# Per-row weights' norm moved into a diagonal product, the steps after it one slot later, and loads spread over the slots of an unrolled attention and FFN program

## What is computed

```python
scores = scale * np.matmul(q, k.transpose(0, 1, 3, 2))
kth = np.partition(scores, -top_k, axis=-1)[..., -top_k:-top_k + 1]   # top_k = 32
scores = np.where(scores >= kth, scores, -1000000000.0)
attn = np.exp(scores - np.max(scores, axis=-1, keepdims=True))
attn = attn / (np.sum(attn, axis=-1, keepdims=True) + 1e-09)
x = np.matmul(attn, v)                      # rows of 8 heads x 64
h = x @ w_in;  y = (h - np.tanh(h)) @ w_out            # first FFN, 512 -> 2048 -> 512
h = y @ w_in2; g = np.where(h > 0, h, np.exp(np.minimum(h, 0)) - 1); out = g @ w_out2
```

## Time and profile before

| | |
|---|---|
| median of 3 runs | 1504.14 us |
| the profiled execution: its own time | 1504.16 us |
| its span, first to last instruction | 1502.3 us |
| mean granted TensorE clock | 0.911 |
| busy: PE, PEld, DVE, ACT, POOL | 1220.8, 1016.0, 849.9, 773.3, 623.1 us |
| chain that ended last | PE 36%, POOL 28%, issue 26%, ACT 4%, DVE 2% |

### The profile page before, as it was taken

The page is one execution under the profiler, slowest core; times in us unless marked ns, Lnnn a source line. Parts: engine busy times, 40 slices in busy tenths (PEclk is TensorE's granted clock), DMA queues, the critical chain, the costliest instruction groups (busy, mean ns, idle before and its releaser), DMA issues.

```text
span 1502.3 us, 21851 instructions
## 1 busy us (share of the span) xinstructions
PE 1220.8 (81%) x7448; PEld 1016.0 (68%) x7448; DVE 849.9 (57%) x1796; ACT 773.3 (51%) x1792; POOL 623.1 (41%) x968
## 2 busy tenths in 40 slices
PE   1455577878877878888678888788999999999998
PEld 1344456657666667777566777677778888888887
DVE  4667776757878657877667788740442222222221
ACT  3456556656667656766665666653532222222221
POOL 1256535555545545544555545444522222222222
PEclk9855679989999879999898999999999999999999
DMA  8200002100001110001110000002410100101000
GB/s 264 74 12 12 7 20 60 43 25 16 12 26 51 51 34 15 12 26 31 52 55 9 27 13 14 18 29 71 148 63 0 56 1 21 36 1 42 1 29 14
DMA packets 45853, 55.93 MB, mean 37 GB/s; under 512 B 9136, under 2 KB 26544, under 8 KB 45744
## 3 DMA queue, kind: packets, MB, share of 16 engines
q1 hardware_dynamic: 45744, 54.55, 11.7%
HBM read 45.09 MB, written 9.44 MB: 36 GB/s over the span
## 4 chain that ended last, share of the span: by engine, by line
PE 36%; POOL 28%; issue 26%; ACT 4%; DVE 2%; SPq 2%; DMA 1%; POOLq 0%; ACTq 0%
PE ps L544 13%; PE ps L527 13%; POOL gT_lo L907 6%; POOL scores L898 6%; POOL gT_raw L902 5%; POOL qT_lo L861 3%; PE ps L497 3%; PE ps L464 2%; POOL kT_hi_over_lo L868 2%; POOL weight_sum_eps L893 2%; PE ps L447 1%; POOL xT_lo L880 1%; POOL exp_bias L886 1%; PE ps L483 1%; PE ps L436 1%
## 5 line engine op out<-in xcount | busy, mean ns | idle before, releaser
L776 DVE MAX8 best<-work 128x8 f32<-128x576 f32 x432 | 309.2, 744 | 0.2
L447 PE MATMUL ps<-ident,scores 128*128 128x128 f32 x576 | 107.9, 318 | 206.9 <-POOL scores L898 206.8
L447 PEld LDWEIGHTS ps<-ident,scores 128*128 128x128 f32 x576 | 74.8, 161 | 225.5 <-POOL scores L898 225.4
L950 POOL TENSOR_TENSOR elu_lo<-elu_h,elu_hi 128x512 fp32r<-128x512 f32 x72 | 92.9, 1290 | 317.6 <-ACT elu_hi L580 317.6
L785 DVE MATCH_REPLACE8 work<-best,work 128x576 f32<-128x576 f32 x288 | 214.0, 743 | 0.0
L907 POOL TENSOR_TENSOR gT_lo<-gT_raw,gT_hi 128x256 fp32r<-128x256 f32 x144 | 109.8, 762 | 200.3 <-ACT gT_hi L580 200.3
L836 DVE TENSOR_SCALAR exp_h<-exp_h 128x512 f32<-128x512 f32 x72 | 30.7, 427 | 269.6 <-ACT exp_h L728 269.6
L902 POOL TENSOR_TENSOR gT_raw<-gT_raw,tanh_h 128x256 f32<-128x256 f32 x144 | 106.1, 737 | 179.2 <-ACT tanh_h L647 178.8
L580 ACT ACTIVATE weights_T<-ps 128x512 f32<-128x512 f32 (+1 forms) x288 | 107.9, 428 | 131.5 <-PE ps L448 131.5
L483 PE MATMUL ps<-xT_hi,w_in_hi 128*128 128x256 f32 x576 | 165.8, 288 | 1.6 <-ACT weights_T L580 1.6
L602 ACT ACTIVATE scores<-ps 128x576 f32<-128x576 f32 x144 | 92.2, 641 | 143.0 <-PE ps L437 142.9
(11 more groups left out here) (73 smaller groups left out, 3083.7 us busy)
## 6 DMA issues: line engine op xcount, KB each, us to landing
kT_raw<-kT SPq DMA_DIRECT2D x64, 144.0 KB, 2.8
qT_raw<-qT SPq DMA_DIRECT2D x128, 64.0 KB, 2.2
w_in_raw<-w_in SPq DMA_DIRECT2D x8, 1024.0 KB, 6.6
w_out_raw<-w_out SPq DMA_DIRECT2D x8, 1024.0 KB, 7.2
ffn_rows<-y_rows SPq DMA_DIRECT2D x18, 256.0 KB, 2.0
v_rows<-v SPq DMA_DIRECT2D x16, 256.0 KB, 3.0
rows<-ffn_rows SPq DMA_DIRECT2D x4, 1024.0 KB, 5.9
out<-out_rows SPq DMA_DIRECT2D x16, 256.0 KB, 2.5
```

The lines of the kernel that those rows point to most:

```text
L447: pe.transpose(ps[:, B_TURN, c * P:(c + 1) * P], w[:, c * P:(c + 1) * P], ident[:, :])
L776: nc.vector.max(best[:, u.t % 3, 1 + n * EIGHT:1 + (n + 1) * EIGHT], src).then_inc(done, 1)
```

## The change

- `norm` is gone. POOL multiplies a 128x128 matrix of ones on the diagonal (kept as bytes) by the inverse (`set_diag`), in the same memory as the identity, and `turn_weights` is an ordinary product of the weights with that diagonal matrix.
- `invert`, `set_diag`, the turn and `copy_turned` come one slot later, in u+3. `invert` stands behind the first MAX8 of its slot. `attend` stands behind the turn of the same slot and ahead of `y_step`. `copy_scores` still reuses the buffer of the unit 4 before it, so it now waits for the turn of its own slot.
- The order within ScalarE's and POOL's slots is written anew: `copy_x` first and `copy_scores`, `copy_turned` behind `tanh_step`; on POOL `difference` first and `sum_eps`, `biases` behind the low parts.
- The weights' loads are issued one in each second slot (2 to 16), each after a wait on `scored`. At the start only one q and one k are split ahead of the slots; the low parts of the first batch's other k come to POOL, in two halves as all k do; the slots of k for later batches change.
- `y_rows` gets a buffer for each of 4 tiles, in the memory of the high part of x; both copies of a group's end stand together, and an x tile waits for its buffer's save.
- For the 21 chunks from EARLY = 123 on (they run when the attention is over) DVE makes the difference straight from PSUM, and the low part, in place of ScalarE's copy and two POOL operations.
- Of the second FFN's weights a quarter is split before it and three quarters beside its first 12 steps (before: three quarters and a quarter).

The diff's core. Renames, semaphores, sizes and waits with the same meaning are left out.

```diff
@@ -95,6 +95,8 @@
+    EARLY = sum(s <= T + 2 for s in h_slot)
@@ -115,12 +117,14 @@
+    K_AFTER = (1, 2, 4, 6, 8, 9, 10, 12)
+    K_FIRST = {-1: (1, 2), 0: (3,), 1: (4,), 2: (5,), 3: (6,), 4: (7,)}
-            k_slot[first + 1 + h * 11 // 7] = (b, h)
+            k_slot[first + K_AFTER[h]] = (b, h)
@@ -156,21 +160,24 @@
+        diag = ident
+        ones_at = place("diagonal_ones", [P, P], U8)
+        y_rows = place("y_rows", [P, KC, RING * P], offset=xt_at)
-        y_rows = place("y_rows", [P, DM])
...
@@ -256,7 +265,7 @@
         def rest_bank(u):
-            return B_H + next_chunk(u.t + 3) % 2
+            return B_H + (next_chunk(u.t + 3) + 1) % 2
@@ -268,6 +277,8 @@
+        w_load_slot = {2 * i + 2: i for i in range(2 * FB)}
@@ -285,13 +296,14 @@
-        w2_in_at, w2_out_at = {}, {}
-        for fb in range(FB - 1):
-            for n in range(CPB):
-                w2_in_at.setdefault(4 * fb + 6 + n // 2, []).append(fb * KC + n)
-                w2_out_at.setdefault(4 * fb + 8 + n // 2, []).append(fb * CPB + n)
-        w2_in_late = {f: [(FB - 1) * KC + 2 * f, (FB - 1) * KC + 2 * f + 1] for f in (0, 1)}
-        w2_out_late = {f: [(FB - 1) * CPB + 2 * f - 4, (FB - 1) * CPB + 2 * f - 3] for f in (2, 3)}
+        w2_in_at = {6: (0, 1), 7: (2, 3)}
+        w2_out_at = {8: (0, 1), 9: (2, 3)}
+        w2_in_late, w2_out_late = {}, {}
+        for fb in range(1, FB):
+            for n in (0, 1):
+                c = fb * CPB + 2 * n
+                w2_in_late[4 * fb - 4 + n] = (c, c + 1)
+                w2_out_late[4 * fb - 2 + n] = (c, c + 1)
@@ -334,6 +346,7 @@
             def load_weights(i):
+                sp.wait_ge(scored, 2 * i + 3)
@@ -374,8 +388,6 @@
-            for i in range(2 * FB):
-                load_weights(i)
@@ -383,18 +395,22 @@
+                if s in w_load_slot:
+                    load_weights(w_load_slot[s])
...
@@ -439,13 +456,16 @@
             def turn_weights(u):
-                pe.wait_ge(normed, u.t + 1)
+                pe.wait_ge(diag_set, u.t + 1)
-                after(pe, tanh_done, next_chunk(u.t + 3) - 1)
+                after(pe, tanh_done, next_chunk(u.t + 3))
-                    pe.transpose(ps[:, B_TURN, c * P:(c + 1) * P], w[:, c * P:(c + 1) * P], ident[:, :])
-                pe.transpose(ps[0:REST, rest_bank(u), REST_AT:BANK], w[:, FULL * P:S], ident[:, :]).then_inc(turned, 1)
+                    pe.matmul(ps[:, B_TURN, c * P:(c + 1) * P], w[:, c * P:(c + 1) * P], diag[:, :],
+                              start=True, stop=True)
+                pe.matmul(ps[0:REST, rest_bank(u), REST_AT:BANK], w[:, FULL * P:S], diag[:, :],
+                          start=True, stop=True).then_inc(turned, 1)
@@ -475,7 +495,8 @@
-                after(pe, turned_copied, min(h_slot[i] - 3, T - 1) + 1)
+                after(pe, g_done_late, i - 1 - EARLY)
+                after(pe, turned_copied, min(h_slot[i] - 4, T - 1) + 1)
@@ -486,12 +507,15 @@
             def y_step(i):
-                pe.wait_ge(g_split, i + 1)
-                if f == 0:
-                    after(pe, y_copied, g * GN)
+                if i < EARLY:
+                    pe.wait_ge(g_split, i + 1)
+                else:
+                    pe.wait_ge(g_split_late, i + 1 - EARLY)
+                    if f == 0 and g > 0:
+                        pe.wait_ge(y_copied, (g - 1) * GN + j + 1)
@@ -545,17 +570,16 @@
...
             for s in range(-1, LAST + 1):
-                done, old, new = unit(s - 3), unit(s - 2), unit(s + 1)
-                if done and done.ends_pair:
-                    attend(done)
+                exped_u, new = unit(s - 3), unit(s + 1)
-                if old:
-                    turn_weights(old)
+                if exped_u:
+                    turn_weights(exped_u)
+                if exped_u and exped_u.ends_pair:
+                    attend(exped_u)
...
@@ -636,24 +660,28 @@
             def x_high_part(tile):
-                after(sc_e, h_done, ((seq_of[tile] - RING) // GN + 1) * FC)
+                after(sc_e, y_saved[seq_of[tile] % RING], seq_of[tile] // RING * DMA)
             def tanh_step(i):
-                high(gt_raw[:, i % 2, :], ps[:, B_H + i % 2, 0:N])
+                if i < EARLY:
+                    high(gt_raw[:, i % 2, :], ps[:, B_H + i % 2, 0:N])
...
             def copy_y(g, j):
-                after(sc_e, y_saved, (g * GN + j) * DMA)
-                high(y_rows[:, :], ps[:, B_Y + j, :]).then_inc(y_copied, 1)
+                high(y_rows[:, :, x_columns(tiles[g * GN + j])], ps[:, B_Y + j, :].rearrange("p (c n) -> p c n", c=KC)
+                     ).then_inc(y_copied, 1)
@@ -671,43 +699,42 @@
-            for n in range(QRING):
-                q_high_part(n)
-                if n == 0:
-                    k_high_part(0, 0)
-                k_high_part(0, n + 1)
+            q_high_part(0)
+            k_high_part(0, 0)
             for s in range(-1, LAST + 1):
-                new, old, done = unit(s + 1), unit(s - 2), unit(s - 3)
+                new, old, exped_u, done = unit(s + 1), unit(s - 2), unit(s - 3), unit(s - 4)
+                if done and done.ends_pair:
+                    copy_x(done)
-                if new:
-                    copy_scores(new)
-                if y_in.get(s - 1, 0) % FC == FC - 1:
-                    copy_y(y_in[s - 1] // FC, 0)
-                    copy_x(done)
-                for n in q_load_slot.get(s - 1, ()):
+                if y_in.get(s - 1, 0) % FC == FC - 1:
+                    for j in range(GN):
+                        copy_y(y_in[s - 1] // FC, j)
+                if s in h_in:
+                    tanh_step(h_in[s])
+                if new:
+                    copy_scores(new)
+                if exped_u:
+                    copy_turned(exped_u)
+                if 0 <= s < QRING - 1:
+                    q_high_part(s + 1)
+                for n in q_load_slot.get(s, ()):
-                if 0 <= s and s + 4 < H:
-                    k_high_part(0, s + 4)
+                for h in K_FIRST.get(s, ()):
+                    k_high_part(0, h)
-                if s in h_in:
-                    tanh_step(h_in[s])
-                if old:
-                    copy_turned(old)
-                if y_in.get(s - 1, 0) % FC == FC - 1:
-                    copy_y(y_in[s - 1] // FC, 1)
@@ -728,6 +755,9 @@
+                    if g == 0 and f == 0:
+                        for n in range(RING):
+                            sc_e.wait_ge(y_saved[n], (TILES - n + RING - 1) // RING * DMA)
@@ -788,32 +818,45 @@
 ...
+            def difference(i):
+                ve.wait_ge(tanh_done, i + 1)
+                after(ve, y_done, i - 1)
+                nc.vector.tensor_tensor(gt_raw[:, i % 2, :], ps[:, B_H + i % 2, 0:N], gt_tanh[:, i % 2, :], ALU.subtract
+                                        ).then_inc(g_done_late, 1)
+            def g_low_part(i):
+                ve.wait_ge(g_high, i + 1)
+                nc.vector.tensor_tensor(gt_lo[:, i % 2, :], gt_raw[:, i % 2, :], gt_hi[:, i % 2, :], ALU.subtract
+                                        ).then_inc(g_split_late, 1)
-            for h in range(PAIRS):
-                k_low_part(0, h)
+            k_low_part(0, 0)
             for s in range(-1, LAST + 1):
-                new, old, exped_u = unit(s), unit(s - 1), unit(s - 2)
+                new, old, exped_u = unit(s), unit(s - 1), unit(s - 3)
+                if exped_u:
+                    invert(exped_u)
-                if exped_u:
-                    invert(exped_u)
-                if 0 <= s and s + 4 < H:
-                    k_low_part(0, s + 4)
+                if h_in.get(s - 1, -1) >= EARLY:
+                    g_low_part(h_in[s - 1])
+                if h_in.get(s, -1) >= EARLY:
+                    difference(h_in[s])
@@ -861,12 +904,14 @@
-            def k_low_part(b, h, t):
-                po.wait_ge(k_high, b * H + h + 1)
-                po.wait_ge(summed, t - 1)
-                nc.gpsimd.tensor_tensor(z[D:P, h, :], z_raw[D:P, h, :], k_up[D:P, :], ALU.subtract).then_inc(k_split, 1)
-                po.wait_ge(k_split, b * H + h + 1)
+            def k_low_part(b, h, half, before, count):
...
+                nc.gpsimd.tensor_tensor(z[D:P, h, cs], z_raw[D:P, h, cs], k_up[D:P, cs], ALU.subtract).then_inc(k_split, 1)
+                po.wait_ge(k_split, n * 2 + half + 1)
@@ -883,19 +928,19 @@
...
+            def set_diag(u):
-                w = sc[:, u.t % 4, :]
-                nc.gpsimd.tensor_scalar(w, w, rinv[:, u.t % 2:u.t % 2 + 1], 1.0, ALU.mult, ALU.mult).then_inc(normed, 1)
+                after(po, turned, u.t)
+                nc.gpsimd.tensor_scalar(diag[:, :], ones_at[:, :], rinv[u.t % 2], None, ALU.mult).then_inc(diag_set, 1)
@@ -910,39 +955,54 @@
-            for n in range(QRING):
-                q_low_part(n)
+            q_low_part(0)
             for s in range(-1, LAST + 1):
-                old, exped_u, done = unit(s - 1), unit(s - 2), unit(s - 4)
```

(49 more changed lines are left out.)

86 lines of the change are left out of this document (56 added, 30 removed).

## The result

Four runs of the changed kernel took 1428.03 us (median; 1426.44 to 1432.71), four of the kernel before, run in turn with them, 1505.12. The ratio is 0.9496, 95% interval 0.9468 to 0.9524. The forecast of 1339 was wrong by 89 us, outside its range: of the 165.6 us forecast, 77 came.

The account below looks back on a forecast made before the run. Waits were taken to set the attention slots, with PE 98% busy in the second FFN; after the change PE's pair of 11.3 us stood above DVE's 4.9 a slot. Stage terms summed to -165.6 from 1504.16: 1339 us, range 1300 to 1375.

Parts of the forecast that it names:

- the turn as an ordinary product: PE's turn of the weights: 0.1 us a product, bounds 0.06 and 0.24, or -0.2 to +0.65 us a slot.
- rival 3: The turn's product takes four passes: 0.24 us each, 0.65 us in some 132 slots, +86, 1425 us; chance 0.06.
- Start -21.9: Start to five slots done: 38.7 instead of 60.6 us, without ACT's 18.18 us wait for q and 3.7 earlier.
- 23 slots -36.7: Slots to the first chunk at the fourth last: 15 at 4.9, 4 at 5.65, 4 tails; 122.5 against 159.2 us.
- k -73.0: Three stretches of 16 slots with k: 93.0 us each, against 116.3, 119.0 and 116.7.
- 20-slot stretches -8.7: Two stretches, each 16 slots at 5.65 and 4 tails at 7.1: 118.8 us against 123.9 and 122.4.
- After the attention -15: 22 slots after the attention at PE's 2.95 us, chunk chain shortened on DVE: 68.6 against 83.6 us.
- The good slots gain nothing: Slots without the start's, biases' or k's waits: 11.3 us a pair after the change against 11.2, bounds 11.0 to 11.9.
- Rival 2: Each 1 MB weight load delays a q; the first stretch gives back about 36 us, 1375; chance 0.08.
- Rival 1: Spread k still lengthens its slots through ACT; the 73 us stay away, 1412 us; chance 0.14.
- Rival 4: PE's new wait at `attend` lowers its clock between slots 24 and 143; 1606 us at 30 pairs; chance 0.04.
- Rival 5: ACT is ready ahead and slots without a tail run at DVE's 4.9 us; 71 less, 1268 us; chance 0.06.

Follow-up runs that it names:

- with transposes: The changed kernel with the turn as transposes against the identity again and POOL's norm of the weights one slot later than before the change; 1336.16 us, ratio 0.8872.
- the kernel with both edits: The changed kernel with transposes and the late norm put back, and `attend` moved to the head of the next slot; 1256.25 us, ratio 0.8342.

## Why the prediction was wrong, and where it was right

**The step that failed** is "the turn as an ordinary product: I take 0.1, as the transposes and near to `attend`". It measured 0.245 a product of 128 columns and 1.34 us a turn, 0.84 more than the 0.5 of the sum. The evidence lay in the earlier trace rows: `attend`'s row says x16, for a unit pair whose code has 8 such products. I took these 16 and 4 for products of 64 weight columns, put two side by side for one of 128, and divided 1.39 us by ten; they are 8 + 2 products, each issued twice. A comparison of that count with the code would have shown it: ten products, two side by side, are five in 1.39 us, 0.28 each, near the 0.245. (Whether two halves do run side by side no run shows; without that, ten products in 1.39 us are 0.14 each, and the price of 128 weight columns stays open.) The tail's row was misread in the same way, which changed nothing in the sum. The kernel's fp32r products, `y_step` and `h_step`, stand one row for each product.

With the product taken back, the sum holds: 1336.16 measured against 1338.6. Stage by stage in the table, the column with transposes stays within 5.3 us of the forecast, and a pair is 10.92 against 11.3 (just below the bound of 11.0, which left out ACT's lateness). That the total comes within 2.5 us is in part luck: the start and the last 27 slots came 9 us shorter than forecast, the stage after the last scores 5 us longer, and in the slots with k the shorter pair made up for slots that were longer than the sum had (below).

**The upper bound had it.** The end of 0.24 a product, +86 us and 1425 (rival 3, 0.06) is the measured 1428, though hardly by its reasoning: the 0.24 came from `y_step`, 512 columns of another type, and the profile counts two instructions of 0.12; how many passes each makes no run shows. So the near hit of 1425 is luck in its source. I had the bound and took the other end, and the range of 1300 to 1375 counted the product's lower bound but not its upper. What decided for 0.1 was the misread row of `attend`.

**The page.** The Trainium skill, "TensorE: Matmul & The Clock Gate", section Terms, has transpose mode four times faster for FP32; by that I had worked out 1537. Here four transposes take 0.43 us and four fp32 products 0.98, 2.3 times as long. The measurement decides: a rule that I put aside on a misread row pointed the right way, at less than its full size. The Trainium skill, "Perfetto Trace Analysis", section Engine Utilization, halves TensorE's output rate for FP32_LOW_HIGH; it doesn't say which products are of that kind. The doubled count of instructions would be in line with it, but no run shows that the turn's products are, nor what each of the two instructions does.

**Term by term.**
- Start -21.9: -24.5 (60.6 to 36.1). Right, and 18.3 of it are the loads alone.
- 23 slots -36.7: -30.8; with transposes -36.0. Right but for the product.
- k -73.0: -40.1; with transposes -71.3. Right in mechanism: in the changed kernel the first two stretches are 2.8 us longer than 16 slots of a good pair (6.44 us a slot against 6.26), about the 2.6 that the sum had; the third is 5.9 longer. With transposes the three are 4.7, 6.3 and 7.5 us longer than 16 slots of 5.46; they meet the forecast since a good pair is 0.38 us shorter than the 11.3. Not foreseen was how much depends on POOL's subtraction standing behind the diagonal.
- 20-slot stretches -8.7: **+16.6**, and the last 27 -10.3: **+7.4**. Here nothing else was to be had, and the sign is the product's. With transposes -12.9 and -15.2.
- After the attention -15: **-6.6**. A second error. These rows are the first `h_step` behind the last `attend` and the first `h2`, in the kernel before and in the changed one:

```profile
1009.75 0.28 PE L483 MATMUL ps<-xT_hi,w_in_hi 128*128 128x256 f32 x1
...
1086.10 0.63 PE L527 MATMUL ps<-yT_hi,w_in_hi 128*128 128x512 f32 x1
```

```profile
941.51 0.28 PE L504 MATMUL ps<-xT_hi,w_in_hi 128*128 128x256 f32 x1
...
1007.26 0.39 PE L552 MATMUL ps<-yT_hi,w_in_hi 128*128 128x512 f32 x1
```

  The sum took 68.6 us instead of 83.6 for the 22 slots without a turn (the first begins at 1009.75 and at 941.51 here). They are 65.8, better than forecast, but the kernel before had spent 76.4 on them and not 83.6, a figure that no row has: -10.6. From the last scores to there it is 26.1 us instead of 23.0, +3.1, and this stretch still holds four turns (with transposes it is 22.9 us, so the 3.1 are the product's), and the second FFN is 0.9 longer. With transposes the stage gives -9.7.
- `set_diag` "between 0.2 and 0.75, I take 0.35": 0.61, off the path, as said.
- "The good slots gain nothing": right with transposes (10.9 against 11.2), and with the product they lose 1.3 us a pair.

**The rivals.** Rival 2 (q meets the weights) did not come: the one longer wait for q is at the start. Rival 1 (spread k lengthens its slots) did not come in the changed kernel, whose slots of 7.73 us are at most 8.1 for k's sake. It came in part in the kernel with transposes, where ACT copies two heads of k in slots that follow each other and comes late:

```profile
221.84 1.09 PE L482 MATMUL ps<-weights_T,v_rows 128*64 128x128 f32 x16 [2.74 <-issue]
```

PE waits 2.74 us there, and the slot takes 8.29 us instead of 7.04. Rival 4 (the clock falls) did not come at its size: with 1.49 us of waiting in each second slot the granted clock is 0.95 to 1.00 in the stages behind the first 23 slots, as the earlier trace rows had it; single slots at a lower clock take 9.3 us instead of 7.7. With transposes it is 0.93 from 100 to 500 us, which the sum did not have either. With the order on POOL undone it fell behind some waits of 1.4 us, and not behind others. Rival 5 (DVE's 4.9) is what the kernel with both edits comes near to, at 1256.25 against 1268, for which the `attend` wait had to vanish: there it was made to.

## What to carry to other kernels

Before an operation is priced by a neighbour's row, the count in that row is to be held against the number of calls in the code; where the count is double, the row's time belongs to half as many products. A scaling folded into a matrix product has to be priced with the product's type: here a late `norm` on an engine with room was as good as the fold in fp32r (which rounds the weights), and the fold in plain fp32 cost 92 us. And when the bound moves to another engine, the small orders (which of two copies comes first) have to be tried again, since their sign can turn.

## What the runs showed of the hardware that was not expected

- A product of plain fp32 is two instructions in the profile (576 products, 1152 rows): one of 128 columns takes 0.245 us, against 0.11 for the fp32 transpose and 0.10 for the fp32r product.
- POOL's multiply of 128 byte columns into fp32 takes 0.61 us, nearly as much as 0.75 for 576 fp32 columns (late norm: 749 ns on average). This is not a fixed part alone: POOL's addition of EPS on one fp32 column takes 0.22 us, and its one plain copy of the same 128 byte columns into fp32 0.29. What makes the multiply of bytes slow no run shows.
- A wait of 1.37 us at the turn was followed by a slot at a granted clock of 0.68 that took 2.9 us longer; a wait of 1.39 us in the same kernel was followed by a slot at 1.00.
